# The second MLP's Strassen products added up in PSUM, its weights split on the core as they are used

## The reference

```python
def _moe_ref(x, w1, w2, w3, w_out):                 # 3072 tokens, 512 -> 768 -> 512
    h = np.maximum(np.maximum(x @ w1, x @ w2), x @ w3)
    return (h @ w_out).astype(np.float32)

def _moe2_ref(x, w_in, w_out):                      # 3072 tokens, 512 -> 2048 -> 512
    h = x @ w_in
    beta = 1.0
    neg = h <= -beta
    pos = h >= beta
    g = np.where(pos, h, np.where(neg, 0.0, (h + beta) ** 2 / (4.0 * beta)))
    return (g @ w_out).astype(np.float32)

def reference(**kwargs):
    ...
    attn_out = _attn_ref(**attn_kwargs)
    B, H, S, D = attn_out.shape
    x = np.ascontiguousarray(attn_out.transpose(0, 2, 1, 3)).reshape(B * S, H * D)
    x = _moe_ref(x=x, **moe_kwargs)
    return _moe2_ref(x=x, **moe2_kwargs)
```

## Time and profile before

| | us |
|---|---|
| median of three runs (983.39 to 983.95) | 983.58 |
| the profiled execution's own time | 983.69 |
| its span in the trace | 981.6 |
| TensorE busy | 968.8 (99%) |
| VectorE busy | 469.6 (48%) |
| ScalarE busy | 354.5 (36%) |
| GpSimd busy | 150.0 (15%) |

### The profile page before, as it was taken

One profiled execution on the slowest core, in us unless ns is written; L12 is line 12 of the kernel. 1 busy time (PEld: TensorE's weight loads), 2 busy tenths in 40 slices (PEclk: granted clock), 3 DMA queues, 4 the chain that ended last, 5 costly groups with the idle time before them and its releaser, 6 DMA issues.

```text
span 981.6 us, 18566 instructions
## 1 busy us (share of the span) xinstructions
PE 968.8 (99%) x7968; PEld 905.1 (92%) x7968; DVE 469.6 (48%) x713; ACT 354.5 (36%) x553; POOL 150.0 (15%) x176
## 2 busy tenths in 40 slices
PE   6999999999999999999999999999999999999998
PEld 5999999999999999999998888988888888888887
DVE  4662524244252434425456655566545666454452
ACT  3342212222222222222353625545354544444253
POOL 2022442405235230000000000000000000000000
PEclk9999999999999999999999999999999999999999
DMA  9462753645465361042735566655756545575532
GB/s 363 186 234 70 267 183 128 252 144 188 162 236 183 153 231 61 1 172 65 269 131 217 203 220 215 204 196 200 249 191 236 192 161 196 187 258 170 198 118 108
DMA packets 32206, 181.52 MB, mean 185 GB/s; under 512 B 3456, under 2 KB 7552, under 8 KB 21888
## 3 DMA queue, kind: packets, MB, share of 16 engines
q0 software_dynamic: 9216, 92.28, 27.0%
q1 hardware_dynamic: 22912, 88.09, 24.4%
HBM read 144.70 MB, written 35.65 MB: 184 GB/s over the span
## 4 chain that ended last, share of the span: by engine, by line
PE 98%; DMA 1%; DVE 0%; ACT 0%; issue 0%; SPq 0%
PE mlp_ps L491 23%; PE mlp_ps L492 23%; PE mlp_ps L493 23%; PE attn_ps L493 3%; PE scores_ps L493 3%; PE attn_ps L492 3%; PE scores_ps L492 3%; PE attn_ps L491 3%; PE scores_ps L491 3%; PE attn_ps L484 3%; PE scores_ps L457 2%; PE trans_ps L493 2%; PE trans_ps L492 2%; PE trans_ps L491 1%; PE trans_ps L466 1%; DMA qk_raw<-qk_l 1%
## 5 line engine op out<-in xcount | busy, mean ns | idle before, releaser
L491 PE MATMUL mlp_ps<-x_hi,w_hi 128*128 128x384 f32 x572 | 195.1, 341 | 0.0
L493 PE MATMUL mlp_ps<-x_lo,w_hi 128*128 128x384 f32 x572 | 191.5, 335 | 0.0
L492 PE MATMUL mlp_ps<-x_hi,w_lo 128*128 128x384 f32 x572 | 191.2, 334 | 0.0
L492 PE MATMUL mlp_ps<-yc,wi 128*128 128x384 f32 x448 | 150.7, 336 | 0.0
L493 PE MATMUL mlp_ps<-yc,wi 128*128 128x384 f32 x448 | 149.6, 334 | 0.0
L491 PE MATMUL mlp_ps<-yc,wi 128*128 128x384 f32 x448 | 149.6, 334 | 0.0
L787 ACT ACTIVATE ramp<-up,half_col 128x768 f32<-128x768 f32 x64 | 60.1, 939 | 197.4 <-DVE up L1004 178.2
L491 PEld LDWEIGHTS mlp_ps<-x_hi,w_hi 128*128 128x128 f32 x572 | 107.4, 188 | 1.9
L492 PEld LDWEIGHTS mlp_ps<-x_hi,w_lo 128*128 128x128 f32 x572 | 107.5, 188 | 0.0
L493 PEld LDWEIGHTS mlp_ps<-x_lo,w_hi 128*128 128x128 f32 x572 | 107.4, 188 | 0.0
L492 PEld LDWEIGHTS mlp_ps<-yc,wi 128*128 128x128 f32 x448 | 84.1, 188 | 8.8
(11 more groups left out here) (138 smaller groups left out, 1653.0 us busy)
## 6 DMA issues: line engine op xcount, KB each, us to landing
wi<-wi_scratch POOLq DMA_DIRECT2D x32, 1792.0 KB, 7.5
wo<-wo_scratch POOLq DMA_DIRECT2D x32, 1024.0 KB, 5.1
qk_raw<-qk_l SPq DMA_DIRECT2D x24, 768.0 KB, 8.1
wi_scratch<-stage_a SPq DMA_DIRECT2D x8, 1792.0 KB, 8.2
v_raw<-v_l SPq DMA_DIRECT2D x24, 512.0 KB, 4.8
wo_scratch<-stage_a SPq DMA_DIRECT2D x8, 1024.0 KB, 6.6
y_scratch<-y_stage SPq DMA_DIRECT2D x32, 192.0 KB, 2.6
y_raw<-y_scratch SPq DMA_DIRECT2D x8, 768.0 KB, 5.3
```

Source lines behind the costliest of these rows:

```text
L491: pe.matmul(out_ap, a_hi, b_hi, start=first, stop=False, skip_group_check=beside)
L492: pe.matmul(out_ap, a_lo, b_hi, start=False, stop=False, skip_group_check=beside)
L493: return pe.matmul(out_ap, a_hi, b_lo, start=False, stop=last, skip_group_check=beside)
```

## The change

**Products.** Another form of the same scheme (seven products, with sums made one upon another). Three products begin a sum in a bank, four add to what lies in it (`begins`, matmuls that don't clear the bank). A bank is read out by ScalarE or VectorE between two products that add up in it. Every product but two is now copied by ScalarE (`copied` counts five a period, product 3 into a new tile `m5`), and VectorE adds three times (`folded` counts three a period) on 128x384 each.

**Weights.** `w_in` and `w_out` of a pair are loaded as they are (512 KB each) in every period. VectorE makes four sums of 128x256 (`weight_sums`), GpSimd copies to the high parts (`high_in`, casts of 1024 and 768 columns; `high_out`, a cast of 1024), VectorE subtracts to the low parts (`weight_lows`, 1024 and 768 columns; `out_weight_low`, 1024). The work for w_in of period g + 1 stands in period g. The preparation beside phase A, the two DRAM copies and SP's loads and stores for them are gone. There is one buffer for the raw w_in and one for the raw w_out. For g = 0 the sums and low parts stand in the last tile of phase A, at f = 4 and f = 5.

**Activations.** Four sums of 384 columns a half instead of one of 768 and three of 384, in another order. The low parts are as many columns as before, and in every window of a period.

**ScalarE's order.** Copying product 6 and the relu of half 1 come first in a period, the square of half 1 after the copy of product 0, and the two `g_high` together behind it. The unit's `copy_out` are placed otherwise.

The core of the diff:

```diff
+W_S1, W_A11, W_A12, W_A22, W_S2, W_S3, W_S4 = range(7)
+Y_B11, Y_T3, Y_B21, Y_B22, Y_T1, Y_T2, Y_T4 = range(7)
+PRODUCTS = ((W_A11, Y_B11), (W_A12, Y_B21), (W_S2, Y_T2), (W_S1, Y_T1), (W_S3, Y_T3), (W_S4, Y_B22), (W_A22, Y_T4))
...
+            def high_in(g):
+
+                w = wi[g % 2]
+                if g == 1:
+                    pool.wait_ge(mlp_done, TG * (TILES - 1) + L1G)
+                elif g:
+                    pool.wait_ge(prod_done, 7 * (g - 1))
+                pool.wait_ge(w_sums_done, 4 * g + 2)
+                pool.tensor_copy(w[:, :, 0, 0:4 * P], w_raw[:, :, :, :].rearrange("p j x c -> p j (x c)")).then_inc(w_hi_done, 1)
+                pool.wait_ge(w_sums_done, 4 * g + 4)
+                pool.tensor_copy(w[:, :, 0, 4 * P:7 * P], w_sums[:, :, :, :].rearrange("p j x c -> p j (x c)")).then_inc(w_hi_done, 1)
+            def high_out(g):
+
+                pool.wait_ge(wo_raw_in, 16 * (g + 1))
+                if g >= 2:
+                    pool.wait_ge(down_done, SUBS * (g - 1))
+                pool.tensor_copy(wo[:, g % 2, 0], wo_raw[:, :, :]).then_inc(wo_hi_done, 1)
...
+            for g in range(PERIODS):
+                if g + 1 < PERIODS:
+                    high_in(g + 1)
+                high_out(g)
+                if g + 2 < PERIODS:
+                    pool.wait_ge(w_split, 2 * (g + 2))
+                    load_w(g + 2)
+                if g + 1 < PERIODS:
+                    pool.wait_ge(wo_split, g + 1)
+                    load_wo(g + 1)
...
-                elif i < 2:
-                    pe.wait_ge(folded, 6 * (g - 1) + 5 + i)
-                elif i < 5:
-                    pe.wait_ge(copied, 3 * g + i - 1)
+                elif i == 0:
+                    pe.wait_ge(folded, 3 * g)
+                elif i == 1:
+                    pe.wait_ge(copied, 5 * g)
+                elif i == 2:
+                    pe.wait_ge(copied, 5 * g + 1)
+                elif i == 3:
+                    pe.wait_ge(folded, 3 * g + 1)
                 else:
-                    pe.wait_ge(folded, 6 * g + i - 2)
+
+                    pe.wait_ge(copied, 5 * g + i - 2)
                 if i == 0:
-                    pe.wait_ge(wi_in[g % 2], 16 * (g // 2 + 1))
+                    pe.wait_ge(w_split, 2 * (g + 1))
...
+            COPY_TO = {0: (0, 0), 2: (0, 1), 4: (1, 1), 6: (1, 0)}
...
+            def weight_sums(g):
+
+                a21, a11, a12, a22 = (w_raw[:, :, i] for i in range(4))
+                s1, s2, s3, s4 = a21, w_sums[:, :, 0], w_sums[:, :, 1], w_sums[:, :, 2]
+                dve.wait_ge(w_raw_in, 16 * (g + 1))
+                dve.wait_ge(w_split, 2 * g)
+                for i, (o, a, b, op) in enumerate(((s3, a11, a21, ALU.subtract), (s1, a21, a22, ALU.add),
+                                                   (s2, s1, a11, ALU.subtract), (s4, a12, s2, ALU.subtract))):
...
+            def weight_lows(g):
+
+                w = wi[g % 2]
+                for i, (part, src) in enumerate(((slice(0, 4 * P), w_raw), (slice(4 * P, 7 * P), w_sums))):
+                    dve.wait_ge(w_hi_done, 2 * g + i + 1)
+                    dve.tensor_tensor(w[:, :, 1, part], src[:, :, :, :].rearrange("p j x c -> p j (x c)"),
+                                      w[:, :, 0, part].bitcast(F32), ALU.subtract).then_inc(w_split, 1)
+
+            def out_weight_low(g):
+                dve.wait_ge(wo_hi_done, g + 1)
...
             for g in range(PERIODS):
                 if g:
-                    fold(g - 1, 6)
                     g_values(g - 1, 0)
                     g_values(g - 1, 1)
+                fold(g, 0, 0)
+                if g:
                     g_low(g - 1, 0)
-                first_difference(g)
-                if g:
                     g_low(g - 1, 1)
-                less_m5(g)
+                if g + 1 < PERIODS:
+                    weight_sums(g + 1)
                 yc_work(g, 0)
-                fold(g, 3)
                 yc_work(g, 1)
-                fold(g, 4)
+                if g + 1 < PERIODS:
+                    weight_lows(g + 1)
+                fold(g, 1, 1)
                 yc_work(g, 2)
-                fold(g, 5)
+                fold(g, 0, 1)
+                out_weight_low(g)
```

More of the change, by code:

```diff
@@ L194, in build_attention_and_two_mlps @@
         y_stored = [sem(f"y_stored{d}") for d in range(KD)]
[L196 to L199, removed]
+        w_raw_in, w_sums_done, w_hi_done, w_split = sem("w_raw_in"), sem("w_sums_done"), sem("w_hi_done"), sem("w_split")
+        wo_raw_in, wo_hi_done, wo_split = sem("wo_raw_in"), sem("wo_hi_done"), sem("wo_split")
         y_in = [sem(f"y_in{j}") for j in range(2)]
@@ L398, in split_w_out @@
-            def split_w_out(n):
-                p = n // 2
-                raw = stage_b[:, n % 2]
-                hi, lo = w_both[:, 0:WO_COLS].bitcast(F32R), w_both[:, WO_COLS:2 * WO_COLS].bitcast(F32R)
-                pool.wait_ge(raw_in[1], 16 * (p + 1))
-                pool.wait_ge(w_split, 3 * n)
-                pool.wait_ge(w_stored, 16 * n)
-                pool.tensor_copy(hi, raw).then_inc(wo_hi_done, 1)
-                pool.wait_ge(wo_hi_done, p + 1)
-                for i in range(2):
-                    part = slice(i * DM, (i + 1) * DM)
-                    pool.tensor_tensor(lo[:, part], raw[:, part], hi[:, part].bitcast(F32), ALU.subtract).then_inc(w_split, 1 + i)
@@ L749, in _, with yc_high @@
                 tile_a(2 * b + 2, 0)
-            def yc_high(v, j):
+            def yc_high(v, j, parts):
                 if v >= 2:
@@ L788, in bent, with squared @@
                                scale=0.5).then_inc(ramp_done, 1)
-                if between is not None:
-                    between()
+            def squared(g, f):
                 act.wait_ge(ramp_done, 2 * g + f + 1)
@@ L809, in _ @@
                 if g:
+                    copy_product(g - 1, 6)
                     bent(g - 1, 1)
@@ L812, in _ @@
                 if g:
+                    squared(g - 1, 1)
                     g_high(g - 1, 0)
-                copy_product(g, 1)
-                if g:
                     g_high(g - 1, 1)
+                if u and p == 1:
+                    for s in range(2, 5):
+                        copy_out(u - 1, s)
                 copy_product(g, 2)
@@ L820, in _ @@
                     y_out(TILES - 1, 2 * g + 1)
+                if u and p == 1:
+                    copy_out(u - 1, 5)
+                copy_product(g, 3)
+                if u + 1 < TILES_B and p in (2, 5):
+                    yc_high(u + 1, p // 5, HI_ORDER[0:2])
+                copy_product(g, 4)
+                if u + 1 < TILES_B and p in (2, 5):
+                    yc_high(u + 1, p // 5, HI_ORDER[2:4])
                 if u and p == 0:
@@ L823, in _ @@
                         copy_out(u - 1, s)
-                if u and p == 1:
-                    for s in range(2, SUBS):
-                        copy_out(u - 1, s)
-                if u + 1 < TILES_B and p in (2, 5):
-                    yc_high(u + 1, p // 5)
                 bent(g, 0)
+                squared(g, 0)
             g = PERIODS - 1
-            bent(g, 1, lambda: g_high(g, 0))
+            copy_product(g, 6)
+            bent(g, 1)
+            g_high(g, 0)
+            squared(g, 1)
             g_high(g, 1)
@@ L936, in yc_sum @@
                 n = 2 * v + j
+                (b11, b12), (b21, b22) = ((y_raw[:, j, h, 0], y_raw[:, j, h, 1]) for h in range(2))
+                t1, t2, t4 = (y_sums[:, i * TT:(i + 1) * TT] for i in range(3))
                 if k == 0:
```

232 lines of the change are left out of this document (83 added, 149 removed).

## The result

The changed kernel took 993.03 us (median of four runs, 992.61 to 993.76). The kernel before took 983.77 us (four runs, 983.39 to 984.41). The ratio is 1.0092, with a 95% interval from 1.0079 to 1.0104. The forecast was 992.4 us. The profiled execution of the changed kernel is the slowest of its four: 993.76 us, with a span of 991.6.

A forecast was written before the change was run, and what follows sets the result against it. TensorE, busy for 99% of the span, was taken to bound the kernel. Unit stalls of 7.2 us and 1.55 at phase B's start, on a span of 981.6 with 2.09 outside it, gave 992.4 us; range 985.0 to 998.0.

The forecast's parts named there:

- What bounds the kernel: TensorE, busy 99% of the span, with instructions as many and as large as before; only its waits can move.
- Mutual exclusion and its price: GpSimd's casts and VectorE operations with two SBUF inputs run one at a time; the one that waited saves about 0.14 us.
- handovers: Six switches between VectorE and GpSimd in a lap's queue, each hiding 0.14 us: 6.89 becomes 6.05 us.
- Full price: Rival: handovers hide nothing, a lap is 0.84 us longer, a unit 4.2; 1005 us, chance 0.08.
- Cover is enough: Rival: casts and VectorE don't exclude each other or handovers cost less; only 1.55 us remains, 985.2 us, chance 0.15.
- An ordinary lap: Cycle from one period's last fold to the next without yc_work: 14.44 us, under the 15.64 period, costing TensorE nothing.
- Laps with yc_work: Periods 2 to 6 of the first three units: yc_work adds 10.0 us, 82.2 against 78.2; 2.4 us stalls a unit.
- The room at the start: Undisturbed, the last fold is usable by TensorE 1.62 us before product 0 needs it, absorbing part of the 4.0 excess.
- The start of phase B: Products (0, 0) +0.75, (0, 5) +0.1, (0, 6) -0.3 and (1, 1) +1.0 us: together 1.55.
- Removed parts, loads, ScalarE's copies, end of the program: Removed preparation and stores, smaller phase B loads, new copies in gaps, and the last unit's chain: all put at nothing.
- The sum: 7.2 us of unit stalls and 1.55 at phase B's start: 8.75 us more, giving 992.4 us.

The follow-up runs named there:

- the extra cast: Changed kernel with GpSimd's first cast of a period (1024 columns) done twice: 1007.75 us, 1.0245 times the kernel before.
- both moves: Changed kernel with all yc_work behind the last fold on VectorE, and three reorderings where phase B begins: 983.78 us, 1.0001 times the kernel before.

## Why the prediction was right, step by step

**What bounds the kernel.** TensorE's own work, unchanged. Right: its pace is 0.173 us in every kernel here (but for the stretches of lower clock with the extra cast, last section), and with both moves its span is before's.

**Mutual exclusion and its price.** Right, and it carries the forecast. The three handovers of an ordinary period save 0.14 or 0.15 each, as the one row of phase A showed. Full price would have been 1005; the extra cast cost 0.83 us a lap for its 1.04. "Cover is enough" (985.2) is what the kernel does when the exclusion is taken away (985.6 to 986.4 in the experiments without weights' work or with memsets), so that rival had its time right and its condition wrong.

**An ordinary lap.** Worked out at 14.44, measured 14.54 behind the `yc_work` of the second and third unit and 14.7 in the period shown, under 15.64: no stall. Half of the 0.24 more in the period shown lies in the queue: 6.17 us from the third sum (618.47) to where the last fold could end (624.64), where 6.05 was worked out. The other half lies ahead of it, 8.51 (609.96 to 618.47) for 8.39.

**Laps with yc_work.** From last fold's end to last fold's end in the first unit, in us:

| p | 2 | 3 | 4 | 5 | 6 | sum |
|---|---|---|---|---|---|---|
| worked out (14.44 and the `yc_work`) | 16.44 | 17.04 | 15.84 | 17.14 | 15.74 | 82.2 |
| measured | 16.41 | 17.00 | 15.80 | 17.08 | 15.73 | 82.0 |

The room at the start was 1.62 as said (the fold of p = 1 ended at 498.14, product 0 of p = 2 started at 499.82), so 82.0 - 78.2 - 1.6 = 2.2 us of stall a unit. The places are as said (product 0 of p = 4 to 7, the longest at p = 6 with 1.31, none in the last unit), but p = 5 and p = 7 have 0.13 and 0.08 only. 2.4 us a unit in the forecast and 2.25 measured, 7.2 against 6.76 in all: the term was 0.4 too large. That each lap came out within 0.06 is partly luck. The lap beneath was 0.1 too short (14.44 for 14.54), and `yc_work` was too dear, 10.0 for the 9.3 that it adds to five laps of 14.54. The two errors nearly cancel in each lap; neither touches the mechanism.

**The start of phase B.** Forecast 1.55, measured 1.83. Product (0, 0) +0.75 became 0.78 + 0.08, product (0, 5) +0.1 became 0.19, product (0, 6) -0.3 was -0.28, product (1, 1) +1.0 became 0.95 + 0.11. What the forecast didn't count is in each of them: the matmul behind a delayed one comes another 0.08 to 0.11 late. The same holds for the late starts of before, and it could have been read there (the product after the wait lasted 1.15).

**Removed parts, loads, ScalarE's copies, end of the program.** All put at nothing. The kernel with both moves bears them out together: 1.0001 (0.9992 to 1.0010).

**The sum.** 8.75 us forecast, 8.6 by the starts in the traces, 9.26 between the medians. Of the 0.6 between the last two, 0.2 are the small lateness of later matmuls, and the rest isn't a matter of phase B. The trace of the changed kernel is longer by 1.2 us ahead of product (0, 0), and its execution is the slowest of the four. In the eight experiments, whose phase A has the same instructions up to its last tile, that product was due between 463.97 and 466.51 us, with before at 465.25 in the middle of them. The 25 runs of the kernel before, made beside the later experiments, lie as far apart (982.13 to 985.08). So the 1.2 us lie within what executions differ by, and need no cause in the change.

The traces show where they come from, the first 40 us. The same 64 small matmuls of the first tile, in before and then with the cast of w_out moved, whose product (0, 0) was due first of all:

```profile
17.36 1.93 PE L484 MATMUL mlp_ps<-prob_t,v_raw 64*64 64x32 f32 x64
...
17.46 1.13 PE L436 MATMUL mlp_ps<-prob_t,v_raw 64*64 64x32 f32 x64
```

The trace's records of the granted clock begin with a stretch at 1.00 (2.4 GHz), and it begins at 17.4 us of the span in the second of these, at 26.5 in before and at 28.5 in the changed kernel. Matmul number 600, counted from 0, starts at 37.68, 39.23 and 40.18 us, and from there to product (0, 0) the ten traces differ by no more than 0.3. Ahead of their first record the view prints 1.00 too, so the "granted clock of 1.00 throughout" of before holds from 26.5 us on. What decides when the clock rises is left open.

## What to carry to other kernels

When work is put on VectorE and GpSimd together, add up their times as one queue wherever GpSimd reads SBUF and VectorE reads two inputs from it, and hold the sum against the period, not each engine's share of busy time: here 59% and 17% busy stopped TensorE. Then look at what stands ahead of the one instruction that the bound engine waits for. Work that is not needed for it belongs behind it: two reorderings, with no instruction taken away, gave back the whole 9 us.

## What the runs showed of the hardware

**Reading excludes, writing doesn't.** The fourth sum takes 1120 ns on average beside casts of GpSimd, 426 beside memsets of as many columns, 426 with the casts on ScalarE.

**A restart costs about 0.1 us beyond the wait.** A matmul of 384 columns that had to wait is followed by the next at 0.25 to 0.29 us instead of 0.173, in the changed kernel's twelve late products of the units.

**TensorE's clock fell after three of four waits of about 2 us.** The changed kernel, whose latest product in the units was 1.31 us late, has a granted clock of 1.00 throughout phase B. With the extra cast, the product at 532.94 was 2.07 us late, and the granted clock (PEclk in the windows below) fell to 0.57 on average, near the lower of its two levels, 1.2 of 2.4 GHz:

```profile
core 0: us, PE busy (x) PEld busy (x) DVE busy (x) ACT busy (x) POOL busy (x), PEclk, DMA share, GB/s
528.00:532.00 4.00, 3.03 (x16) 2.45 (x14) 4.00 (x5) 0.00 (x0) 1.66 (x2) 1.00 0.00 0
532.00:534.00 2.00, 1.06 (x4) 1.06 (x5) 2.00 (x3) 1.05 (x2) 0.00 (x0) 0.79 0.64 186
534.00:537.00 3.00, 3.00 (x10) 2.56 (x9) 0.98 (x2) 2.92 (x5) 0.53 (x1) 0.57 0.51 180
537.00:540.00 3.00, 3.00 (x16) 2.69 (x15) 2.65 (x4) 1.82 (x3) 0.00 (x0) 1.00 0.11 45
```

The starts of matmuls of 384 columns then stand 0.32 us apart, and 0.17 again from 537.04 on:

```profile
532.94 0.52 PE L445 MATMUL mlp_ps<-yc,wi 128*128 128x384 f32 x1 [1.90 <-DVE up L986]
533.26 0.52 PE L446 MATMUL mlp_ps<-yc,wi 128*128 128x384 f32 x1
```

This came once in each unit and took about 1.5 us of TensorE's time, after products that were 2.07, 2.07 and 2.16 us late; one other that was 2.07 late (at 797.80) and those of 1.74 and less had no such stretch. What it cost the kernel depended on what stood behind it. In the first and second unit it fell into the lap of p = 4, which took 16.81 and 16.80 us, against 16.64 in the third unit, where the clock stayed: 0.2 us, since VectorE went on while TensorE was slow and the next waits were shorter. In the third unit it fell behind product (22, 0), the last long wait of that unit. The periods of p = 6 and 7 are longer there by 1.68 and 0.00 us, against 0.93 and 0.11 in the second unit: 0.6 us.
